# A fused linear-attention, MLP and expert-attention kernel: the third unit's q and k are prepared later, expert slots are reordered, and output products move a slot forward

## What is computed

```python
# 1: complex diagonal linear attention, a = a_re + i a_im, normalised to |a| <= 0.999
for t in range(S):
    S_re, S_im = (ar * S_re - ai * S_im) + k[t] v[t]^T, ar * S_im + ai * S_re
    y[t] = q[t] @ S_re
# 2: MLP on x (768 x 384 per batch item): relu, 3-tap convolution over tokens, sigmoid gate
h = relu(x @ w_in);  h = h * sigmoid(conv3(h));  x = h @ w_out
# 3: four attention experts (head size 64), causal, the top 2 of 4 by a gate
for e in range(4):
    a = softmax(causal(q_e @ k_e^T / 8));  ye = a @ v_e @ wo[e]
    out += gate[e] * ye
```

## Time and profile before

| what | value |
|---|---|
| median of 3 runs | 810.47 us (810.45 to 812.06) |
| the profiled execution, its own time | 814.83 us |
| its span, first to last instruction | 813.0 us |
| mean granted TensorE clock | 0.969 of full speed |
| TensorE busy | 681.2 us (84%) |
| VectorE busy | 613.6 us (75%) |
| ScalarE busy | 390.4 us (48%) |
| DMA moved | 73.84 MB, mean 91 GB/s |

### The profile page before, as it was taken

One profiled execution on the slowest core, in us unless ns is written; L12 is line 12 of the kernel. 1 busy time (PEld: TensorE's weight loads), 2 busy tenths in 40 slices (PEclk: granted clock), 3 DMA queues, 4 the chain that ended last, 5 costly groups with the idle time before them and its releaser, 6 DMA issues.

```text
span 813.0 us, 13049 instructions
## 1 busy us (share of the span) xinstructions
PE 681.2 (84%) x5160; PEld 509.3 (63%) x5160; DVE 613.6 (75%) x1234; ACT 390.4 (48%) x719; POOL 0.2 (0%) x4
## 2 busy tenths in 40 slices
PE   0025638999988998999978999999988999999997
PEld 0024537776655687876646787776566788777565
DVE  4999996999979568899888387998888365440562
ACT  6403065434746663434756663435645324334564
POOL 0000000000000000000000000000000000000000
PEclk9999767999999999999999999999989999999999
DMA  8384452500056532400076343200155140000001
GB/s 326 161 232 117 118 148 48 193 2 0 1 152 199 158 99 72 163 1 1 0 206 212 96 114 126 88 1 0 40 156 162 55 119 2 1 0 1 1 8 53
DMA packets 95837, 73.84 MB, mean 91 GB/s; under 512 B 10912, under 2 KB 87968, under 8 KB 95136
## 3 DMA queue, kind: packets, MB, share of 16 engines
q1 hardware_dynamic: 95776, 73.01, 29.7%
HBM read 49.34 MB, written 23.65 MB: 90 GB/s over the span
## 4 chain that ended last, share of the span: by engine, by line
PE 52%; DVE 36%; ACT 5%; issue 4%; DMA 2%; SPq 0%; DVEq 0%; ACTq 0%
PE wide L1349 6%; DVE cv L997 5%; PE wide L1245 5%; PE wide L1368 5%; PE wide L1320 5%; PE bank L1419 4%; PE wide L1310 4%; PE wide L1403 3%; DVE m L836 3%; PE wide L1257 3%; PE bank L1427 3%; PE wide L1344 3%; DVE m L835 2%; DVE heads L1001 2%; PE bank L1320 2%
## 5 line engine op out<-in xcount | busy, mean ns | idle before, releaser
L1310 PE MATMUL wide<-x_hi_lo,win_hi 128*128 128x384 f32 x384 | 109.4, 355 | 1.1 <-DVE x_hi_lo L959 1.1
L1320 PE MATMUL wide<-heads,wout 128*128 128x384 f32 x256 | 89.6, 493 | 5.8 <-DVE heads L1001 5.8
L1037 DVE TENSOR_REDUCE nmax<-wide 128x1 f32<-128x768 f32 (+2 forms) x96 | 55.3, 618 | 32.1 <-PE wide L1377 31.8
L643 ACT ACTIVATE xs<-wide 128x896 f32<-128x896 f32 x48 | 44.1, 919 | 69.4 <-PE wide L1403 69.4
L997 DVE SCALAR_TENSOR_TENSOR cv<-h,wconv,cv 128x768 f32<-128x768 f32 x64 | 64.9, 1015 | 13.2 <-ACT cv L596 11.4
L1310 PEld LDWEIGHTS wide<-x_hi_lo,win_hi 128*128 128x128 f32 x384 | 70.4, 190 | 5.6 <-issue 3.0
L1320 PEld LDWEIGHTS wide<-heads,wout 128*128 128x128 f32 x256 | 46.9, 189 | 37.7 <-DVE heads L1001 11.7
L1245 PE MATMUL wide<-heads 96*128 96x128 f32 x384 | 55.5, 305 | 17.7 <-DMA heads<-heads_dram 17.7
L1368 PE MATMUL wide<-attn 64*128 64x512 f32 (+3 forms) x256 | 66.3, 491 | 2.3 <-ACT attn L619 2.3
L1232 PE MATMUL wide<-ident,heads 96*128 96x96 f32 x160 | 19.3, 272 | 56.4 <-DMA heads<-heads_dram 56.4
L1245 PEld LDWEIGHTS wide<-heads 96*128 96x128 f32 x384 | 51.5, 215 | 22.0 <-DMA heads<-heads_dram 18.4
(11 more groups left out here) (138 smaller groups left out, 1380.5 us busy)
## 6 DMA issues: line engine op xcount, KB each, us to landing
heads<-heads_dram SPq DMA_DIRECT2D x96, 192.0 KB, 3.6
araw<-a_in SPq DMA_DIRECT2D x12, 768.0 KB, 6.6
araw<-qk_in SPq DMA_DIRECT2D x12, 768.0 KB, 6.5
heads_dram<-m SPq DMA_DIRECT2D x24, 384.0 KB, 2.8
heads_dram<-araw SPq DMA_DIRECT2D x24, 384.0 KB, 2.9
v<-v_in SPq DMA_DIRECT2D x4, 1536.0 KB, 7.1
out_dram<-h SPq DMA_DIRECT2D x24, 192.0 KB, 2.0
wout<-w_out_t SPq DMA_DIRECT2D x1, 1536.0 KB, 12.2
```

Of the source, the lines that this page charges most:

```text
L643: nc.scalar.activation(probT[:, t % PROBT, :], wide[2][:, 0:KEYS], ACT.Copy).then_inc(s_pc, 1)
L1037: dve.tensor_reduce(nmax[:, t, side:side + 1], slot_scores(t, side), AXX, ALU.max, negate=True).then_inc(s_nm, 1)
L1310: last = MM(low[u % 2][:, 0:NT], w[:, k, mt * P:(mt + 1) * P], xs[:, k, n * NT:(n + 1) * NT], start=(k == 0 and part == 0), stop=(k == KT ...
L1320: last = MM(mlp_bank[u][:, 0:NT], wout[:, mt, k * P:(k + 1) * P], hgate(mt)[:, n * NT:(n + 1) * NT], start=(mt == 0), stop=(mt == MT - 1))
```

## The change

- **VectorE, expert slots.** `row_sums` and `scale_probs` of t + 1 come directly behind `row_max` (t + 2), and the preparing call comes after them. That call is now one operation (`qk_product`, `inverse_first`, `inverse_second`) or `scale_qk`, where it was two operations. The decay moves from slot 9 to slot 10, one `gate_sumsq` from slot 8 to 9.
- **The third unit.** For batches 1 to 3 its `scale_qk` and its four products leave the expert slots of the batch before and stand in chunk 0 of the batch's own linear attention. So its `store_unit` moves too, behind `load_heads(b, 3)`. The unit's `load_a` for the next batch follows that store, and both stand before `load_heads(b, 4)`; in batch 0 only `load_a` moves past `load_heads(0, 4)`.
- **ScalarE.** `squares`, `magnitude`, `ln` and `guess` of the third unit for the next batch move from the end of the experts and chunks 0 and 2 to chunks 3 and 4; `gate_sumsq` on VectorE goes to chunk 4.
- **Output products.** `final` of the short side and its `copy_out` move from slots 7 and 11 to slots 6 and 10. `store_out(b, 1)` now stands before `move_decay`.

```diff
--- before.py
+++ after.py
@@ -485,10 +485,10 @@
                 if b == 0:
                     load_a(1, 1)
                     move_decay(0, 2, 3, 5)
-                    store_unit(0, 2)
+                store_unit(b, UNITS - 1)
+                if more:
+                    load_a(b + 1, UNITS - 1)
                 load_heads(b, 4)
-                if b == 0:
-                    load_a(1, 2)
                 load_heads(b, 5)
                 if more:
                     sp.wait_ge(s_y, NC * b + NC)
@@ -506,12 +506,9 @@
                     if b + 2 < B:
                         load_a(b + 2, 1)
                 store_out(b, 0)
+                store_out(b, 1)
                 if more:
-                    store_unit(b + 1, 2)
-                    if b + 2 < B:
-                        load_a(b + 2, 2)
                     move_decay(b + 1, UNITS - 1, 0, NC - 1)
-                store_out(b, 1)
                 store_out(b, 2)
                 for r in range(2):
                     sp.wait_ge(s_out[r], 16 * NC // 2 * (b + 1))
@@ -661,9 +658,8 @@
                 for c in range(NC):
                     if c + 1 < GAINS:
                         copy_k(b, c + 1)
-                    if b and more and c < UNITS:
+                    if b and more and c < UNITS - 1:
                         if c == 0:
-                            magnitude(b + 1, UNITS - 1)
                             exp_tables()
                         ln(b + 1, c)
                         guess(b + 1, c)
@@ -671,9 +667,14 @@
                         w_squares(0, 2)
                         w_ln(0, 2)
                         w_guess(0, 2)
-                    if b == 0 and c == 4:
-                        magnitude(1, 2)
                     copy_x(b, c)
+                    if more and c == 3:
+                        squares(b + 1, UNITS - 1)
+                    if more and c == 4:
+                        magnitude(b + 1, UNITS - 1)
+                        exp_tables()
+                        ln(b + 1, UNITS - 1)
+                        guess(b + 1, UNITS - 1)
                     if b == 0:
                         if c in (0, 1):
                             squares(1, c)
@@ -684,12 +685,6 @@
                             for u in range(2):
                                 ln(1, u)
                                 guess(1, u)
-                        if c == 3:
-                            squares(1, 2)
-                        if c == 4:
-                            exp_tables()
-                            ln(1, 2)
-                            guess(1, 2)
                 nc.scalar.preload_act_table_set("sigmoid_and_others")
                 for mt in range(MT):
                     if b == 0 and mt == 0:
@@ -736,7 +731,7 @@
                         copy_o(b, t // E - 1, t % E)
                     if t > E and t % E == 1:
                         copy_out(b, t // E - 1, 0)
-                    if t > E and t % E == 3:
+                    if t > E and t % E == 2:
                         copy_out(b, t // E - 1, 1)
                     if b + 2 < B and t in (6, 9):
                         squares(b + 2, t // 3 - 2)
@@ -751,8 +746,6 @@
                     copy_o(b, PAIRS - 1, side)
                 for side in range(2):
                     copy_out(b, PAIRS - 1, side)
-                if b + 2 < B:
-                    squares(b + 2, UNITS - 1)
 
             for side in range(2):
                 act.sem_inc(s_fe[side], 1)
@@ -910,14 +903,21 @@
                 dve.wait_ge(s_wsq, UNITS * b + u + 1)
                 TT(m[:, 0, unit(u)], m[:, 0, unit(u)], m[:, 1, unit(u)], ALU.add).then_inc(s_n, 1)
 
+            def inverse_first(b, u):
+
+                total, y0, t = (m[:, r, unit(u)] for r in range(3))
+                dve.wait_ge(s_r0, UNITS * b + u + 1)
+                TT(t, total, y0, ALU.mult).then_inc(s_rn, 1)
+
+            def inverse_second(b, u):
+
+                y0, t = (m[:, r, unit(u)] for r in (1, 2))
+                dve.wait_ge(s_rn, 2 * (UNITS * b + u) + 1)
+                STT(t, t, 2.0, y0, ALU.subtract, ALU.mult, reverse0=True).then_inc(s_rn, 1)
+
             def inverse(b, u):
-
-                total, y0, t = (m[:, r, unit(u)] for r in range(3))
-                n = UNITS * b + u
-                dve.wait_ge(s_r0, n + 1)
-                TT(t, total, y0, ALU.mult).then_inc(s_rn, 1)
-                dve.wait_ge(s_rn, 2 * n + 1)
-                STT(t, t, 2.0, y0, ALU.subtract, ALU.mult, reverse0=True).then_inc(s_rn, 1)
+                inverse_first(b, u)
+                inverse_second(b, u)
 
             def scale_qk(b, u):
 
@@ -928,7 +928,7 @@
                     part = tiles(araw[:, x, :], u)[:, :, half]
                     TT(part, part, tiles(m[:, 2, :], u)[:, :, half], ALU.mult).then_inc(s_sc, 1)
 
-            def qk_products(b, u, part):
+            def qk_product(b, u, part, x):
 
 
                 n = UNITS * b + u
@@ -936,10 +936,18 @@
                     dve.wait_ge(s_sc, 2 * n + 2)
                 else:
                     dve.wait_ge(s_pr, 4 * n + 2)
+                src = araw[:, x, unit(u)]
+                TT(m[:, x, unit(u)] if part else src, src, (w_im if part else w_re)[:, unit(u)],
+                   ALU.mult).then_inc(s_pr, 1)
+
+            def qk_products(b, u, part):
                 for x in (1, 0):
-                    src = araw[:, x, unit(u)]
-                    TT(m[:, x, unit(u)] if part else src, src, (w_im if part else w_re)[:, unit(u)],
-                       ALU.mult).then_inc(s_pr, 1)
+                    qk_product(b, u, part, x)
+
+            def last_unit(b, part, x):
+
+
+                qk_product(b, UNITS - 1, part, x)
 
             def mask(b, c):
                 for quad in range(2):
@@ -1056,17 +1064,22 @@
                 more = b + 1 < B
                 if b:
                     mask(b, 0)
+                    scale_qk(b, UNITS - 1)
+                    last_unit(b, 1, 1)
                     state_sum(b, 0)
-                    if more:
-                        gate_sumsq(b + 1, UNITS - 1)
                 else:
                     first_chunks()
                 for c in range(0 if b else 2, NC):
                     if c + 1 < NC:
                         mask(b, c + 1)
+                        if b and c == 0:
+                            last_unit(b, 1, 0)
                         state_step(b, c)
                     if c + 1 < GAINS:
                         state_sum(b, c + 1)
+                    if b and c == 0:
+                        last_unit(b, 0, 1)
+                        last_unit(b, 0, 0)
                     if c:
                         x_low(b, c - 1)
                     if b == 0 and c == 2:
@@ -1080,6 +1093,8 @@
                         write_w(1, 0)
                     if b and more and 1 <= c < NC - 1:
                         (norm if c % 2 else write_w)(b + 1, (c - 1) // 2)
+                    if b and more and c == 4:
+                        gate_sumsq(b + 1, UNITS - 1)
                 x_low(b, NC - 1)
                 if more and b == 0:
                     norm(1, 1)
@@ -1128,25 +1143,27 @@
                     for side in range(2):
                         if t + 2 < SLOTS:
                             row_max(b, t + 2, side)
-                    if more:
-                        if t == 0:
-                            qk_products(b + 1, 0, 0)
-                        if t == 1:
-                            inverse(b + 1, 2)
-                        if t in (2, 5):
-                            scale_qk(b + 1, t // 2)
-                        if t in (3, 4):
-                            qk_products(b + 1, 1, 4 - t)
-                        if t in (6, 7):
-                            qk_products(b + 1, 2, 7 - t)
-                        if t == 9:
-                            decay(b + 1, UNITS - 1, 0, NC - 1)
                     if t + 1 < SLOTS:
                         row_sums(b, t + 1)
                         for side in range(2):
                             scale_probs(b, t + 1, side)
-                    if b + 2 < B and t in (8, 11):
-                        gate_sumsq(b + 2, t // 3 - 2)
+                    if more:
+                        if t in (0, 1):
+                            qk_product(b + 1, 0, 0, 1 - t)
+                        if t == 2:
+                            scale_qk(b + 1, 1)
+                        if t in (3, 4):
+                            qk_product(b + 1, 1, 1, 4 - t)
+                        if t in (5, 6):
+                            qk_product(b + 1, 1, 0, 6 - t)
+                        if t == 7:
+                            inverse_first(b + 1, 2)
+                        if t == 8:
+                            inverse_second(b + 1, 2)
+                        if t == 10:
+                            decay(b + 1, UNITS - 1, 0, NC - 1)
+                    if b + 2 < B and t in (9, 11):
+                        gate_sumsq(b + 2, (t - 9) // 2)
 
```

## The result

| what | before | changed |
|---|---|---|
| median | 811.26 us (810.45 to 812.84, 4 runs) | 825.76 us (823.65 to 835.15, 4 runs) |
| the profiled execution, its own time | 814.83 us | 823.65 us |
| its span | 813.0 us | 821.7 us |
| mean granted clock | 0.969 | 0.952 |
| TensorE / VectorE / ScalarE busy | 681.2 / 613.6 / 390.4 us | 683.7 / 613.1 / 395.7 us |

The changed kernel takes 1.0199 of the time before (95% interval 1.0118 to 1.028): slower, though whether by as much as 2% the interval leaves open, and outside the predicted range of 801 to 820. The two profiled executions lie 8.8 us apart, the medians 14.5: the profile of before fell on a long execution, that of the changed kernel on its shortest.

A forecast was written before the change was run, and what follows sets the result against it. VectorE was taken to set the pace of the expert slots in batches 0 to 2. Terms -22.7 - 2.6 + 12.0 + 9.1 + 5.1 = +0.9 us, on a median of 810.47, gave 811.4 us, range 801 to 820.

The forecast's parts named there:

- Slots: Expert slots: less VectorE work per slot and earlier output products gain 22.7 us over four batches (ends 13 and 27).
- 2.6 for the clock: Experts of batches 0 and 2: denser slots spare TensorE low-clock time, a gain of 2.6 us (ends 0 and 5.1).
- The walk: Both engines stepped through the expert slots: last projection to last transposes takes 42.2 us instead of 48.0 in preparing batches.
- Taking 1.5 us off for the stores: Experts of batches 0 and 1: store_out(b, 0) lands late for copy_out, reducing the gain by 1.5 us each.
- The premise: Expert slots, batches 0 to 2: VectorE sets the pace, 4.05 us a slot, 3.19 with one operation of 0.87.
- Third unit's products at no cost: Chunk 0 of the linear attention: the third unit's five calls, 4.4 us, fit where VectorE idles, costing nothing.
- Loads of chunk 4: Linear attention: stores and load_a ahead delay chunk 4's scores, a loss of 12.0 us over four batches.
- the rival: Chunk 4's loads are hardly late, since the queue takes gates and heads side by side: 802.0 us, chance 0.2.
- copy_x of chunk 5: Start of the MLP: copy_x stands behind ScalarE's chain, losing 9.1 us over batches 1 and 2; batch 0 loses 0.
- The clock again: TensorE idle at chunk 4 and before the second h_products brings lower-clock stretches, a loss of 5.1 us (ends 0 and 12).
- the clock turns it slower: Rival: 6.8 us at lower clock, not 3.4, follows each of batches 1 and 2's four idle stretches: 818.2 us, chance 0.2.
- The starting point: Whole kernel: the +0.9 us sum of terms is laid on the median of 810.47 us, not the profiled 814.83.

The follow-up runs named there:

- unit_moved: The kernel before with only the third unit's move (scaling, products, stores, load of gates, ScalarE chain): 847.11 us, ratio 1.0454.
- slots_outputs: The kernel before with sums and scaling directly behind row_max and the short side's final and copy_out a slot forward: 793.92 us, ratio 0.9764.
- chunk_4_off_the_stores: The changed kernel with chunk 4's loads ahead of the third unit's stores, fetching chunk 3's lines instead: 820.01 us, ratio 1.0107.
- gates_load_later: The changed kernel with the third unit's load_a behind the loads of chunk 4: 818.18 us, ratio 0.9999.
- scaling_order_alone: The kernel before with only the sums and scaling directly behind the maxima in each slot: 808.19 us, ratio 0.9927.

## Why the prediction was wrong

The signs and places of all terms were right, if not the reason given for the gain; the wait for chunk 4's loads and the low clock were put too small, and the time they start from was too low. By the marks the terms came to +8.7 us where the sum said +0.9: the loads of chunk 4 were 5.5 short, `copy_x` and the clock behind both waits together 2.1, the slots 0.2. In batches 1 and 2 alone the added waits were 19.0 us where I had 17.1 and the added busy time 10.3 where I had 5.1.

- **Slots.** 22.7 and 2.6 for the clock, 25.3 together; measured 25.1. That is in part luck. The walk gave 42.2 us up to the last transposes in each preparing batch; it was 44.7, 43.5 and 41.6 (48.2 before in batch 1, which I had read as 48.0). The 2.1 behind them were 1.1, 2.0 and 2.0. So the division was rougher than the sum: batch 2 gained 10.2 us, batches 0 and 1 only 6.1 and 6.7. Taking 1.5 us off for the stores was right in sign: ScalarE waited 2.38 us for one in batch 0, and TensorE behind it. The premise failed, that VectorE's amount of work sets the pace of these slots. In unit_moved VectorE has 4.4 us less to do a batch, and A to next S of batches 0 to 2 falls by 1.9 us in all; in slots_outputs it has nothing less to do, and it falls by 18.5. What the runs show to count is the order of the operations in a slot together with the place of the output products.
- **Third unit's products at no cost.** Right: 19.44 us in chunk_4_off_the_stores.
- **Loads of chunk 4.** 12.0 forecast, S to C measured 17.5 (6.7, 5.1, 2.0 and 3.7). The failed steps are "stores landed" 9.6 us after the first issue of chunk 3's loads, which was 10.8 in batch 1 and 10.1 in batch 2 (289.71 to 300.52, 477.98 to 488.07), and from the load of the gates to the scores 7.8, which was 9.3 and 8.5. The 5.2 in it, the path with nothing ahead, is right in batch 3 (5.0). With the gates ahead I allowed 5.2 and 2.0, and it took 8.7 and 7.8; with them behind, in gates_load_later, it still took 6.3 and 5.8. The Trainium skill's page "DMA: Bandwidth & Descriptors" ("Queues, rings and completion order") says that completion is not first in, first out for one issuing engine. The trace of gates_load_later agrees: three of chunk 5's loads landed before the gates that were issued ahead of them, 308.75 to 310.46 against 310.56. What I drew from it for the rival, that chunk 4's loads would then not be held by the gates, does not follow: ahead of them the gates cost 2.9 us.
- **copy_x of chunk 5.** 9.1 forecast with 1.7 of clock, 10.8; H to V measured 11.7 in batches 1 and 2. The chain from magnitude to the copy is 3.88 us, exactly the row's. The waits were well sized: 4.81 us in batch 2, and 3.22 in batch 1, where a fall of the clock had already made TensorE late; in unit_moved it is the other way about, 4.82 and 3.15. No dearer table switch appears: the load is 1.28 and its successor starts 0.01 later, so the 2.66 of the Trainium skill's "ScalarE: Activation LUTs" ("What ACT_TABLE_LOAD costs") is again not seen. Batch 0's zero was 1.2 (a wait of 1.56 us where before it was 0.36).
- **The clock again.** 5.1 forecast. In batches 1 and 2 the low clock went from 3.4 to 33.9 us, and TensorE's busy time grew by 10.3. I took one fall of 3.4 us behind each wait. The falls at the waits of chunk 4 lasted 10.2 and 6.8 us, and those at the start of the MLP 3.4 with 6.7, and 6.8. My rival "the clock turns it slower" is this mechanism. Its 818.2 with the loads' shortfall of 5.5 would have been 823.7.
- **The starting point.** I laid the difference of terms on the median of before. The sum said +0.9 and the pair of profiled executions +8.8; the remaining 6.4 us of the miss (14.4 in all) is above all that one execution was long for its kernel and the other short for its own. The pair itself holds 2.4 us of luck in batch 0 (C to H), without which the terms would have been that much further off.

Still open is why the third unit's stores, issued by 295.68 and 484.09, took 4.8 and 4.0 us more to land (3.6 in the earlier trace rows), and whether the low clock could be had without a wait: neither was isolated. The landings show this much: chunk 3's four loads and the four stores landed one behind another, 0.7 to 1.8 us apart, and the first store 4.1 and 4.6 us after its issue, where in the slots of the earlier trace rows, with no load ahead, it was 2.8.

## What to carry to other kernels

Before work is moved into a stage with idle engines, ask what stands in order behind it: here VectorE had the room, and the loss was in SyncE's queue, where loads waited for stores and each later load inherited the lateness, and in ScalarE's, where four instructions stood ahead of a copy that everything waited for. Price a wait of TensorE as its length plus the slower matmuls behind it, read from low stretches in the profile; over the linear attention and MLP of batches 1 and 2 the second part was half of the first. Of two small edits that remove different waits of one loop, neither may show much alone; try them together before either is dropped.

## Not expected of the hardware

The waits of 6.64 and 5.05 us at chunk 4 came with 10.2 and 6.8 us at 1.2 GHz. Short waits came with a fall or without: in an expert slot the 1.55 us wait had 3.4 us behind it in scaling_order_alone, batch 1, and none in batch 0, and at chunk 4 of batch 3 a wait of 1.91 us had none in the changed kernel and one of 1.82 had 3.4 in gates_load_later. That last pair prices such a fall: C to H is 15.5 us with it and 13.9 without. And kernels with long waits scatter more, with exceptions: the changed kernel by 1.4% and its variants with ten runs by 2.1 to 2.6%, but chunk_4_off_the_stores by 0.9% in 4 runs; slots_outputs by 0.6 to 0.8%, scaling_order_alone by 0.7% in 10 (the kernel before by 1.2% in 23 runs).
